# The order of TensorE's three width arms in an expert pass: 576, 608, 640 becomes 640, 608, 576

## The reference

```python
attn_out = _attn_ref(**attn_kwargs)            # q, k, v: (4, 8, 576, 64)
x = attn_out.transpose(0, 2, 1, 3).reshape(B * S, H * D)     # 2304 tokens of 512
a = x @ w1; b = x @ w2                         # 512 -> 1024
x = (a * b @ w3) @ w_out                       # 1024 -> 512
# experts
logits = x @ w_gate
noisy_logits = logits + log1p(exp(x @ w_noise)) * noise
top2 = the two largest of 8 ; top2_w = softmax over the two
for e in range(8):
    for k in range(2):
        mask = top2[:, k] == e
        h = maximum(x[mask] @ w1[e], 0.0)      # 512 -> 1024
        out[mask] += top2_w[mask, k] * (h @ w2[e])           # 1024 -> 512
```

## Time and profile before

| | |
|---|---|
| three timed runs | 1034.65, 1034.64, 1032.08 us; median 1034.64 |
| the profiled execution | 1032.71 us, of which the trace spans 1030.7 us |
| TensorE matmuls | busy 1014.0 us, 98% of the span |
| GpSimd, VectorE, ScalarE | 51%, 43%, 36% |
| granted TensorE clock | full but for one stretch of 6.85 us near the start |
| fetches of TensorE's program (q8) | 29, 0.48 MB |

### The profile page before, as it was taken

One profiled execution on the slowest core, in us unless ns is written; L12 is line 12 of the kernel. 1 busy time (PEld: TensorE's weight loads), 2 busy tenths in 40 slices (PEclk: granted clock), 3 DMA queues, 4 the chain that ended last, 5 costly groups with the idle time before them and its releaser, 6 DMA issues.

```text
span 1030.7 us, 16726 instructions
## 1 busy us (share of the span) xinstructions
PE 1014.0 (98%) x5934; PEld 932.6 (90%) x5935; DVE 446.0 (43%) x935; ACT 370.1 (36%) x683; POOL 529.8 (51%) x416
## 2 busy tenths in 40 slices
PE   7999999999999999999999999999999999999997
PEld 6999999888989898989898998989898989899895
DVE  6888888773214232433325652222222222222221
ACT  6998988853213132322223413212121212111110
POOL 8698999520000202020202136978788887878752
PEclk8999999999999999999999999999999999999999
DMA  8788886383960101010402175262717163634304
GB/s 175 176 198 200 208 209 164 96 274 116 369 247 1 62 0 62 0 62 0 143 1 73 52 233 167 91 175 71 186 40 212 22 194 71 187 78 140 44 2 51
DMA packets 73986, 124.97 MB, mean 121 GB/s; under 512 B 13377, under 2 KB 30913, under 8 KB 73938
## 3 DMA queue, kind: packets, MB, share of 16 engines
q1 hardware_dynamic: 65218, 104.05, 34.1%
q0 software_dynamic: 8640, 20.00, 9.7%
q10 hardware_dynamic: 80, 0.29, 0.1%
HBM read 78.73 MB, written 36.67 MB: 112 GB/s over the span
## 4 chain that ended last, share of the span: by engine, by line
PE 75%; DVE 1%; issue 0%; POOL 0%; ACT 0%; DVEq 0%; POOLq 0%
PE ps_turn L1714 13%; PE ps_x L1690 10%; PE ps_b L1690 10%; PE ps_x L1779 10%; PE ps_a L1761 9%; PE ps_b L1761 9%; PE ps_small L1714 9%; PE ps_a L1670 2%; PE ps_small L1662 1%; PE ps_turn L1652 1%; PE ps_small L1644 0%; POOL out L1274 0%; PE ps_turn L1802 0%; PE ps_small L1645 0%; DVE y_tile L1455 0%
## 5 line engine op out<-in xcount | busy, mean ns | idle before, releaser
L1217 POOL DMA_INDIRECT expert_rows<-x_rows,slot_idx x36 | 41.7, 1157 | 306.1 <-DVE slot_idx L1590 297.0
L1274 POOL DMA_INDIRECT out<-y_tile,out_rows x40 | 63.2, 1579 | 75.1 <-DVE y_tile L1455 70.9
L1317 ACT CAST xT_high<-ps_a 128x512 fp32r<-128x512 f32 x40 | 23.3, 588 | 188.8 <-PE ps_a L1670 188.8
L1392 ACT COPY prod<-ps_a 128x384 f32<-128x384 f32 x48 | 23.1, 481 | 162.1 <-PE ps_b L1761 162.1
L1597 DVE TENSOR_TENSOR prod<-ps_b,prod 128x384 f32<-128x384 f32 x48 | 26.8, 558 | 123.9 <-ACT prod L1392 123.9
L1690 PE MATMUL ps_b<-xT_high,w_high 128*128 128x256 f32 (+3 forms) x256 | 77.5, 303 | 0.0
L1690 PE MATMUL ps_x<-xT_high,w_high 128*128 128x256 f32 (+3 forms) x256 | 76.9, 300 | 0.0
L1690 PE MATMUL ps_x<-xT_low,w_high 128*128 128x256 f32 (+3 forms) x256 | 76.8, 300 | 0.0
L1690 PE MATMUL ps_x<-xT_high,w_low 128*128 128x256 f32 (+3 forms) x256 | 76.8, 300 | 0.0
L1690 PE MATMUL ps_b<-xT_high,w_low 128*128 128x256 f32 (+3 forms) x256 | 76.8, 300 | 0.0
L1690 PE MATMUL ps_b<-xT_low,w_high 128*128 128x256 f32 (+3 forms) x256 | 76.8, 300 | 0.0
(11 more groups left out here) (272 smaller groups left out, 3011.4 us busy)
## 6 DMA issues: line engine op xcount, KB each, us to landing
spare<-e_w SPq DMA_DIRECT2D x16, 1024.0 KB, 5.3
w_raw<-e_w SPq DMA_DIRECT2D x16, 1024.0 KB, 8.4
expert_rows<-zeros SPq DMA_DIRECT2D x8, 1290.0 KB, 15.9
ex_rows<-expert_rows SPq DMA_DIRECT2D x40, 258.0 KB, 3.9
k_raw<-kT SPq DMA_DIRECT2D x31, 288.0 KB, 4.8
out<-zeros SPq DMA_DIRECT2D x11, 512.0 KB, 10.3
q_raw<-qT SPq DMA_DIRECT2D x16, 288.0 KB, 4.6
q_mix<-q_top SPq DMA_DIRECT2D x16, 288.0 KB, 3.8
```

Of the source, the lines that this page charges most:

```text
L1217: nc.gpsimd.indirect_dma_start(out=rows_dram, out_offset=bass.IndirectOffsetOnAxis(ap=slot_idx[:, k, t:t + 1], axis=0), in_=x_rows[:, t, : ...
L1274: nc.gpsimd.indirect_dma_start(out=out, out_offset=bass.IndirectOffsetOnAxis(ap=out_rows[:, j:j + 1], axis=0), in_=y_tile[j][:], in_offset ...
L1317: nc.scalar.copy(xT_high[:, :, j * P:(j + 1) * P], ps_xT[j % XS][:].rearrange("p (c t) -> p c t", t=P)).then_inc(xhigh, 1)
L1392: nc.scalar.copy(prod[f % 2][:], ps_a[f % 2][:, 0:G]).then_inc(a_copied, 1)
```

## The change

The loop that writes the three arms runs over the widths from the last to the first. The program then holds: compare with 2, the arm of 640; compare with 1, the arm of 608; compare with 0, the arm of 576. Each arm is the same as before and still has its own number. Both copies of the body (the loop's and the last stretch's) are written by this one line; the first stretch has no arms. No other engine's program is touched.

```diff
@@ -1734,7 +1734,7 @@
                 pe.wait_ge(weights_cut, 2 * CUTS * before + CUTS)
                 first_product(g, before, 0)
                 step = pe.value_load(widths_i[0:1, bass.ds(g, 1)], min_val=0, max_val=len(WIDTHS) - 1)
-                for k, width in enumerate(WIDTHS):
+                for k, width in reversed([*enumerate(WIDTHS)]):
                     with pe.If(step == k):
                         first_product(g, before, 1, width)
                 pe.wait_ge(weights_cut, 2 * CUTS * before + 2 * CUTS)
```

## The result

The changed kernel takes 1038.54 us (median of 7 runs, 1036.26 to 1040.96), the kernel before 1034.21 us in the same comparison (median of 7, 1032.08 to 1037.24). The ratio is 1.0035 with a 95% interval of 1.002 to 1.005: about 3.6 us slower, 2.1 to 5.2. The forecast was +1.9 us at 1036.5, range 1033.2 to 1038.6. Its place and its sign were right, its size was half of what came, and 1038.54 lies at the very top of the range.

What follows compares the result with a forecast made beforehand. TensorE was taken to bound the kernel end to end. In the last stretch, 2.3 us of wait plus 0.1 refilling less 0.5 for the hole gave +1.9 on 1034.64, so 1036.5 us, range 1033.2 to 1038.6.

Steps and rivals of the forecast that it cites:

- What bounds the kernel, and which arms run: TensorE bounds the last piece end to end; arm 576 runs in stretches 1, 2, 5, 7, arm 608 in 3, 4, 6.
- The last stretch, the wait: Second comparison ahead of the last stretch's arm waits for program text; first matmul starts 2.3 us later, range 2.2 to 2.6.
- block C: Last stretch's program fetch of 987.4, holding the third comparison and third arm; to arrive 3.1 to 3.3 us behind the landing.
- Refilling the queue: Last stretch, behind the wait: refilling TensorE's empty queue of handed-on matmuls adds 0.1 us, range 0 to 0.2.
- The hole's 0.53 us: Last stretch, second product behind the arm: 0.53 us lost after two matmuls in the kernel before, to disappear.
- The clock: Rival: the last stretch's idle time brings half clock for 6.85 us, +3.4 us, in all +5.3, 1039.9; chance 0.09.
- A clock row of 0.50 near 987: Sign in the changed trace's last stretch, half clock (1.2 GHz of 2.4), that would show the prediction failing.
- The first pass: Loop's first pass: second comparison waits for text, hidden because the array has work until 646.98; 0, at most 0.3 us.
- the 0.7 us of the prediction: Assumed time from the event that asks for a program fetch to the start of its packet, about 0.7 us.
- 1910 ns comparison: Long comparison behind the first pass's arm in the kernel before; already hidden, so taking it away gives nothing.
- The later passes, and the page of the Trainium skill: Loop passes 2 to 6 cost 0 as all text stays; rival from the page, two blocks kept: 1043.3, chance 0.02.
- no change within 0.3%: Outcome for the whole kernel: measured time not told from no change, about 3.1 us; chance 0.80.

Runs made afterwards that it cites:

- last_only: Kernel before with the arms as 640, 608, 576 in the last stretch alone, the loop in the old order; ratio 1.0027.
- early_read: Changed kernel with the width read at the start of the stretch, ahead of first_product's first part; ratio 1.0016 against the kernel before.
- changed_again: The changed kernel once more, unedited, for a second profile and more timed runs; ratio 1.0025 against the kernel before.
- loop_only: Kernel before with the arms as 640, 608, 576 in the loop alone, the last stretch in the old order; ratio 0.9997.
- wait_for_cut: Kernel before, old order, with a wait for GpSimd's third weight cut between first_product's two parts in the last stretch; ratio 1.0071.
- shifted_after: Changed kernel with 83 short matmuls, results unused, ahead of the gated product, moving later text 166 instructions along; 1054.61 us.
- shifted_before: Kernel before with 83 short matmuls, results unused, ahead of the gated product, moving later text 166 instructions along; 1051.80 us.

## Why the prediction was right and where it was not

**What bounds the kernel, and which arms run:** right. Passes 2 to 6 are equal to 0.01 us in both traces. The first stretch, which has no arms, is 1.6 us longer in the changed kernel's trace, by the clock's fall at 579.

**The last stretch, the wait:** right in place and cause, too short. Forecast 2.3 us (2.2 to 2.6), measured 2.97. The mis-sized term is the arrival of block C. It was to be 3.1 to 3.3 us behind the landing; it took 984.84 to 988.42, 3.58 us. The runs with this wait gave 3.1 to 3.6: `last_only` 3.3, `early_read` 3.1, `changed_again` 3.6. The packet started 1.26 us behind the landing here and 0.75 in `last_only`, `early_read` and `changed_again`, where 0.7 was assumed. I took the smallest of few samples because it came from the same place in the program.

**Refilling the queue:** 0.1 us was added, and that was right. In `early_read`, with full clock, the second matmul behind the gap starts 0.25 us after the first (985.62 to 985.87) where 0.147 is usual, so 0.10 lost; gap and refilling, 1.66 + 0.10, are the whole of 54.43 - 52.67 = 1.76. In the changed kernel, at half clock, that distance is 0.43 in place of 0.267, so 0.16.

**The hole's 0.53 us:** gone, as forecast. The last stretches that lost nothing put it at 53.17 - 52.67 = 0.50.

**The clock:** this was the rival with a chance of 0.09, and it came true beside the forecast, in every profile in which the long wait left a gap of 2.5 us or more. A clock row of 0.50 near 987 was also one of the prediction's own signs of being wrong, and it is there at 988.47. Working it out: the last stretch lost 57.09 - 52.67 = 4.42 us against a loss-free one, of which 2.97 are the gap, 0.16 the refilling, and 1.3 the half clock (11 matmuls at 0.267 us in place of 0.147). The rival's price, +3.4 us for 6.85 us of half clock, was that of the earlier trace rows; half clock lasted 3.4 us here and 6.8 in two other runs (`last_only` paid 5.55 against 52.67). The step that failed was the argument against it, that TensorE is full ahead of the gap and behind it. That didn't protect the clock.

**The first pass:** forecast 0, at most 0.3; measured 0.49 at the gap and 0.10 of refilling in the changed kernel, 0.43 and 0.10 in its second profile, none in `loop_only`. Another 0.2 us lie at 644.6, where a group starts late with no comparison near; the likely cause is its wait for VectorE to have freed a buffer. The block came 2.7 us behind its packet, close to the 2.3 to 2.6 of the forecast. But already the first comparison waited (1221 ns), not the second, so its target was not yet in the text that was there. The rows of before hint at that: the packet at 658.0, less the 0.7 us of the prediction, was asked for at 657.3, more than 1 us or some 15 instructions ahead of the second comparison at 658.4. By that the second comparison lay in the later block, where the prediction had it just ahead of that block. Whether the count was off by so much or text is wanted so far ahead, no run tells. The forecast had 0.1 to 0.4 us of slack there. That the 1910 ns comparison behind the arm was hidden holds for the kernel before to about 0.05 us; in two other profiles of the old order (`last_only`, `wait_for_cut`) it took 2155 and 2170 ns and 0.3 us were lost.

**The later passes, and the page of the Trainium skill:** the comparisons stay at 68 to 222 ns, and there is no fetch in the changed kernel between 680 and 975. A pass of the loop runs 720 recorded instructions and skips two arms of 201, so the loop has about 1,120, over four blocks of 255. The rule of two blocks in the Trainium skill, "Runtime: NRT & Kernel Launch", "Instruction fetch mechanics", doesn't hold for it. The same section gives TensorE room for 2048 instructions, which this loop would fit in; with that the trace agrees. That a taken branch out of the two blocks forces a fetch before execution goes on, as the section also says, is seen only where the target had not been fetched at all (3521 ns at 984.9).

**The chances and the range:** 0.80 was given to no change within 0.3%, and the measured 0.35% is just beyond it, with an interval that holds both. The median is 0.06 us below the upper end of the range, which had been stretched partly into the clock's case; that it fell inside is luck as much as judgement. The steps of the sum that failed are the wait, +2.3 where 2.97 came, and the clock, left out of it, which cost 1.3. With both, the sum would have been 3.0 + 0.2 + 1.3 - 0.5 for the last stretch and 0.5 for the first pass, +4.5 us. The timed runs gave +3.6 (2.1 to 5.2) and +2.6 (1.0 to 4.1), so the profiles show rather more than the typical run pays. Of the timed runs only the mean clock of the whole execution is on record, so whether it falls behind the gap in all of them stays open.

## What to carry to other kernels

Where a program branches over long arms, count where the arms lie in the blocks in which the text is fetched: a jump over one arm costs the sequencer 0.2 us, and a second jump right behind it, into a block that is asked for only at the first landing, costs it about 3 us or more. It matters only in text that runs for the first time, and only as far as the queue of handed-on work runs out; the order of the arms, the code's length ahead of them and the time at which the deciding number is read all move it. Price idle time of TensorE of 2.5 us and more with the half clock behind it, even in the midst of dense work: here it came in all five profiles with such a gap, and cost 1.3 to 2.7 us.

## What the runs showed of the hardware

- One program fetch of TensorE is 0.02 MB and about 255 instructions; from the landing that asks for it to the end of the waiting comparison 3.0 to 3.6 us pass. The packet starts 0.7 to 1.3 us behind the landing and takes 0.9 to 1.4, and from its end another 1.4 to 1.5 pass.
- The gap from start to start and what the clock did right behind it, in the profiles: 3.73 us (`wait_for_cut`), half clock for 6.8; 3.09 and 3.08 (the changed kernel twice), 3.4; 2.79 (`last_only`), 6.8; 2.54 (`shifted_after`, first pass), 3.4; 1.78 (`early_read`) and 1.57 (`shifted_before`, first pass), full clock. The gap of 1.06 us just ahead of the experts, which all have between short matmuls, was followed by half clock in four of twelve profiles, at 1.57 us a time. So the length of a gap alone doesn't settle it.
- With 83 matmuls of 64 columns in a row TensorE, until then at full clock, had half clock for 10 and 14 us; the kernel before has full clock there.
- A releaser that the profile names for an idle time can be a bystander: VectorE in `early_read`, ScalarE and VectorE in the changed kernel's chain, where the sequencer was waiting for text.
